# Scan and two feed-forward layers on one core: the narrow tile moves to the front, the opening, the output copies, the weight roundings and the gate's affine step are reordered

## What is computed

```python
# x, f_logit: (2, 6080, 256); lower_bound: (256,)
f = lower_bound + (1.0 - lower_bound) * sigmoid(f_logit)
i = 1.0 - f
for t in range(S):                      # per batch row and channel
    h = f[:, t] * h + i[:, t] * x[:, t]
    y[:, t] = h
# then, on the 12160 tokens, two layers one after the other:
h = x @ w_in                            # (tokens, 256) @ (256, 2048)
g = h - np.tanh(h)                      # layer 2: g = np.maximum(0.01 * h, h)
out = g @ w_out                         # (tokens, 2048) @ (2048, 256)
```

## Time and profile before

| | us |
|---|---|
| median of 3 runs | 2082.29 (2079.81 to 2082.47) |
| profiled execution, its own time | 2082.31 |
| its span, first to last instruction | 2080.5 |
| PE busy | 2020.8 (97%) |
| DVE busy | 1626.4 (78%) |
| ACT busy | 1225.4 (59%) |
| POOL busy | 101.8 (5%) |
| mean granted TensorE clock | 0.995 of full |

### The profile page before, as it was taken

How to read it: one execution, slowest core, us unless ns; L and a number is a source line. 1 busy time by engine, 2 the same in 40 slices (tenths; PEclk the granted TensorE clock), 3 DMA queues, 4 the chain that set the end, 5 groups by cost and what they waited for, 6 DMA issues and landing times.

```text
span 2080.5 us, 28416 instructions
## 1 busy us (share of the span) xinstructions
PE 2020.8 (97%) x8700; PEld 1628.8 (78%) x8700; DVE 1626.4 (78%) x2511; ACT 1225.4 (59%) x2168; POOL 101.8 (5%) x101
## 2 busy tenths in 40 slices
PE   6899999999999999999989999999999999999999
PEld 4678778787787877878878778787787877877888
DVE  7888888888888888888787776777777767777676
ACT  4576766766767667676664554544545545455454
POOL 3410000000000000000540000000000000000000
PEclk9999999999999999999999999999999999999999
DMA  3201101101011010010110100101101011010000
GB/s 112 71 31 31 50 14 57 40 20 54 26 40 40 20 60 30 28 58 20 56 64 1 41 21 20 40 0 40 40 0 40 0 40 40 0 40 18 20 21 18
DMA packets 38215, 71.13 MB, mean 34 GB/s; under 512 B 3360, under 2 KB 5920, under 8 KB 38176
## 3 DMA queue, kind: packets, MB, share of 16 engines
q1 hardware_dynamic: 38176, 70.66, 10.1%
HBM read 45.75 MB, written 24.90 MB: 34 GB/s over the span
## 4 chain that ended last, share of the span: by engine, by line
PE 89%; DVE 6%; ACT 3%; issue 2%; DMA 0%; SPq 0%; POOL 0%; ACTq 0%; DVEq 0%
PE y_ps L291 16%; PE y_ps L293 16%; PE y_ps L292 16%; PE x_ps L282 8%; PE x_ps L281 8%; PE x_ps L283 8%; PE q_ps L281 4%; PE q_ps L282 4%; PE q_ps L283 4%; DVE full L702 2%; PE p_ps L281 2%; PE p_ps L282 2%; PE p_ps L283 2%; DVE g_lo L719 1%; DVE part L689 1%
## 5 line engine op out<-in xcount | busy, mean ns | idle before, releaser
L291 PE MATMUL y_ps<-g_hi,wo_hi 128*128 128x512 f32 (+1 forms) x1536 | 610.4, 397 | 29.6 <-ACT y_out L499 18.9
L486 ACT CAST g_hi<-full 128x512 fp32r<-128x512 f32 (+1 forms) x768 | 473.1, 617 | 260.7 <-DVE full L702 135.2
L293 PE MATMUL y_ps<-g_hi,wo_lo 128*128 128x512 f32 (+1 forms) x1536 | 605.8, 394 | 0.0
L292 PE MATMUL y_ps<-g_lo,wo_hi 128*128 128x512 f32 (+1 forms) x1536 | 602.5, 392 | 0.0
L719 DVE TENSOR_TENSOR g_lo<-full,g_hi 128x512 fp32r<-128x512 f32 (+1 forms) x768 | 511.0, 686 | 116.1 <-ACT g_hi L486 110.9
L451 ACT COPY part<-x_ps 128x512 f32<-128x512 f32 (+1 forms) x576 | 334.2, 580 | 267.7 <-PE x_ps L283 257.7
L291 PEld LDWEIGHTS y_ps<-g_hi,wo_hi 128*128 128x128 f32 x1536 | 288.6, 188 | 108.5 <-ACT y_out L499 26.0
L293 PEld LDWEIGHTS y_ps<-g_hi,wo_lo 128*128 128x128 f32 x1536 | 289.4, 188 | 67.7
L292 PEld LDWEIGHTS y_ps<-g_lo,wo_hi 128*128 128x128 f32 x1536 | 288.8, 188 | 61.8
L281 PE MATMUL x_ps<-x_hi,wi_hi 128*128 128x512 f32 (+1 forms) x768 | 301.8, 393 | 24.0 <-POOL wi_lo L831 14.7
L282 PE MATMUL x_ps<-x_lo,wi_hi 128*128 128x512 f32 (+1 forms) x768 | 303.9, 396 | 0.0
(11 more groups left out here) (51 smaller groups left out, 1710.5 us busy)
## 6 DMA issues: line engine op xcount, KB each, us to landing
y<-y_out SPq DMA_DIRECT2D x22, 512.0 KB, 2.8
raw<-y SPq DMA_DIRECT2D x22, 512.0 KB, 4.1
out<-y_out SPq DMA_DIRECT2D x22, 512.0 KB, 2.8
gate<-f_logit SPq DMA_DIRECT2D x40, 256.0 KB, 2.7
drive<-x SPq DMA_DIRECT2D x40, 256.0 KB, 2.9
wi_stage<-w_in SPq DMA_DIRECT2D x16, 256.0 KB, 3.2
wo_stage<-w_out SPq DMA_DIRECT2D x16, 256.0 KB, 2.9
y_out<-f_logit SPq DMA_DIRECT2D x4, 256.0 KB, 4.1
```

Source lines behind the costliest of these rows:

```text
L291: nc.tensor.matmul(bank, hi, g_hi[:, g % 2, c, :W], start=start, stop=False, skip_group_check=True)
L292: nc.tensor.matmul(bank, hi, g_lo[:, g % 2, c, :W], start=False, stop=False, skip_group_check=True)
L293: return nc.tensor.matmul(bank, lo, g_hi[:, g % 2, c, :W], start=False, stop=stop, skip_group_check=True)
L486: nc.scalar.copy(g_hi[:, g % 2, c, :W], full[:, c, :W]).then_inc(g_hi_ready, 1)
```

## The change

1. **Narrow tile first.** The 448-token tile is now the first of each layer, tiles 0 and 12; tiles 11 and 23 have 512. Loops and special cases shift by one.
2. **Opening.** ScalarE takes the first three units, rounds the three plain weight blocks of group 0 that need no sum (`first_wi_round`), X11, the fourth unit, then the sums part; the three chain copies of slot 0 stand between the x roundings, in the order T2, copy, T3, T1, copy, X21, X22, copy, T4. PE has its own `first_slot`: X11 waits only for the first part of the weights, and T3 and T1 come ahead of X21. GpSimd splits group 0 in two parts. VectorE's splits follow the same order.
3. **Gate affine on ScalarE.** `forget_gate` is an Identity activation with scale and bias behind each squash; VectorE's line 608 is gone (44 instructions).
4. **Output copies.** The two `drain` of b=0 stand in slot 0 ahead of `bend` of C21 (in layer 2 ahead of `leak`). Those of b=1 stay in slot 1.
5. **Weight roundings.** `wi_round` stands ahead of `bend` of C11; `wo_round` stays after `round_g` of C11. In tile 0 GpSimd's order is `sum_weights(g+2)`, `wi_split(g+1)`, `wo_split(g)`.
6. **SBUF.** `carry` is allocated last and `zeros` before `bound`; `part`, `full`, `g_hi`, `g_lo`, `y_out` and `zeros` then start at multiples of 128 bytes.

The core of the diff (the transfers' addresses go through `tokens`, and the order of loop and written-out tiles follows from point 1):

```diff
-    W_LAST = seq - LAST * BANK
...
+    W_FIRST = seq - LAST * BANK
...
     def width(s):
-        return W_LAST if isinstance(s, int) and s % TILES == LAST else BANK
+        return W_FIRST if isinstance(s, int) and s % TILES == 0 else BANK
+
+    def tokens(t, b):
+        return b * seq if isinstance(t, int) and t == 0 else t * BANK - (BANK - W_FIRST) + b * seq
...
-        carry = sb("carry", [P, 4], F32)
         part = sb("part", [P, 2, 3, BANK], F32)
...
+        zeros = sb("zeros", [P, BANK], BF16)
         bound = sb("bound", [P, KD], F32)
...
-        zeros = sb("zeros", [P, BANK], BF16)
+        carry = sb("carry", [P, 4], F32)
...
+            def first_slot():
+                W = W_FIRST
+                chain, p_bank, q_bank = x_ps[:, 0, :W], p_ps[:, :W], q_ps[:, :W]
+                pe.wait_ge(first_wi_ready, 1)
+                pe.wait_ge(x_ready, 1)
+                product(chain, 0, W11, X11, W, True, False).then_inc(chain_done, 1)
+                pe.wait_ge(wi_ready, 1)
+                pe.wait_ge(x_ready, 2)
+                pe.wait_ge(chain_copied, 1)
+                product(chain, 0, S2, T2, W, False, False).then_inc(chain_done, 1)
+                pe.wait_ge(x_ready, 3)
+                pe.wait_ge(chain_copied, 2)
+                product(chain, 0, S3, T3, W, False, False).then_inc(chain_done, 1)
+                pe.wait_ge(x_ready, 4)
+                product(q_bank, 0, S1, T1, W, True, False).then_inc(q_done, 1)
+                pe.wait_ge(x_ready, 5)
+                product(p_bank, 0, W12, X21, W, True, True).then_inc(p_done, 1)
+                pe.wait_ge(x_ready, 7)
+                pe.wait_ge(chain_copied, 3)
+                product(chain, 0, W22, T4, W, False, True).then_inc(chain_done, 1)
+                pe.wait_ge(c22_ready, 1)
+                product(q_bank, 0, S4, X22, W, False, True).then_inc(q_done, 1)
...
+            def forget_gate(t, i):
+                W = width(t)
+                k = SCAN_ORDER[i] // 2
+                act.wait_ge(squash_ready, 4 * t + i + 1)
+                nc.scalar.activation(
+                    gate[:, i % 2, :W], gate[:, i % 2, :W], ACT.Identity,
+                    scale=gate_scale[:, k:k + 1], bias=gate_shift[:, k:k + 1],
+                ).then_inc(gate_ready, 1)
+
+            def first_wi_round():
+                act.wait_ge(wi_in[0], 16)
+                nc.scalar.copy(wi_hi[:, 0, W22:S1, :], wi_stage[:, 0, 1:4, :]).then_inc(first_wi_hi_ready, 1)
+
+            def first_wi_sums_round():
+                act.wait_ge(sums_w_ready, 1)
+                nc.scalar.copy(wi_hi[:, 0, S1:, :], wi_stage[:, 0, 4:8, :]).then_inc(wi_hi_ready, 1)
...
                 if scans and g in (1, 2, 3, 4):
                     squash(s + 1, g - 1)
-                copy_chain(q, par, 1, W)
+                    forget_gate(s + 1, g - 1)
+                if not begins:
+                    copy_chain(q, par, 1, W)
...
+                if first and g + 1 < GROUPS:
+                    wi_round(g + 1)
+                if isinstance(s, int) and s == LAST and g >= 1:
+                    wi_round(GROUPS + g - 1)
+                if isinstance(s, int) and s == SWITCH and g == 0:
+                    wi_round(2 * GROUPS - 1)
                 if layer == 1:
                     bend(s, g, C11, W)
...
                 if layer == 1:
                     bend(s, g, C22, W)
+                if g == 0 and not first:
+                    drain(s - 1, 0, 0)
+                    drain(s - 1, 0, 1)
+                if layer == 1:
                     bend(s, g, C21, W)
...
                 if layer == 1:
                     bend(s, g, C12, W)
-                if g == 0 and not first:
-                    drain(s - 1, 0, 0)
-                    drain(s - 1, 0, 1)
...
             def slot(s, g):
                 if s == 0:
-                    wo_split(g)
+                    if g + 2 < GROUPS:
+                        sum_weights(g + 2)
                     if g + 1 < GROUPS:
                         wi_split(g + 1)
-                    if g + 2 < GROUPS:
-                        sum_weights(g + 2)
+                    wo_split(g)
```

179 lines of the change are left out of this document (93 added, 86 removed).

## The result

The changed kernel takes **2010.23 us** (median of 4 runs, 2009.69 to 2011.36); the kernel before, run beside it, 2081.59 us (4 runs, 2079.81 to 2082.47). The ratio is 0.9659, with a 95% interval of 0.9642 to 0.9676.

The account below looks back on a forecast made before the run. PE (TensorE) was taken to bound the kernel. From 2080.5 us, - 13.4 - 0.6 + 0.8 - 21.9 - 6.5 - 11.7 gave 2027.2, plus 1.8 outside the span 2029 us, range 2018 to 2049.

Parts of the forecast that it names:

- Step 6: SBUF start places (homes): matmuls on g fall to the x spacing, 2.9 ns each over 24 a slot, gaining 11.7 us.
- the first rival: Moving the SBUF start places gives nothing, all else as forecast: 2041 us; chance 0.27.
- Step 1: Output copies, tiles 1 to 10: earlier b=0 copies cut the waits, stage 837.4 us, a gain of 13.4.
- The term for the third copy: First b=1 output copy, wanted by PE in slot 1: late, taken as 0.2 us a boundary, ends 0 and 0.6.
- Step 2: Output copies, layer 2, tiles 13 to 23: both pairs in time, stage 919.2 us, gain 0.6; tail grows by 0.8.
- Step 3: Opening and tile 0: tile 1 starts at 105 us in place of 126.91, a gain of 21.9 us.
- Step 4: Tiles 11 and 12, at the turn of layers: 167.2 us in place of 173.7, a gain of 6.5 us.
- Step 5: Gate affine moved to ScalarE: costs nothing under 0.5 us of cover; VectorE's freed 0.5 us hidden under PE in loops.
- The homes do nothing: Rival: new SBUF start places leave the matmul spacing as it was, all else as forecast, 2041 us; chance 0.27.
- Tile 0 slow: Rival: tile 0's seven slots take 86 to 90 us in place of 77, total 2041 or 2053 us; chance 0.10.
- More is gained: Rival: GpSimd's work lies beside idle VectorE time, tile 0 at 98, the turn at 162, total 2017 us; chance 0.05.
- the slow rival: Identity needs its own ScalarE table loads, over 2 us for PE in 44 slots, total 2119 us; chance 0.02.

Follow-up runs that it names:

- e1: The changed kernel with carry and zeros allocated at their old places, so part, full, g_hi, g_lo and y_out start 32 bytes further on; 2048.69 us.
- e4: The changed kernel with the two output copies of b=0 back at the end of ScalarE's slot 0; 2032.69 us.
- e16: The changed kernel with ScalarE's weight roundings back at the end of the slot and GpSimd's old order; 2014.42 us.
- e15: The changed kernel with forget_gate back on VectorE in all loops, the opening keeping it on ScalarE; 2013.87 us.
- e2: The kernel before with only carry allocated last and zeros moved ahead of bound; 2042.82 us.
- e3: TensorE alone, groups of 60 matmuls with varied operand starts and columns, moving blocks 2176 bytes apart; within 228.3 to 234.3 ns a matmul at 512 columns.
- e8: TensorE alone, 24 groups of 60 matmuls with varied operand places, most moving blocks 64 to 160 bytes short; within 228.3 to 234.3 ns at 512 columns.
- e11: TensorE alone, with cases where moving operand and weights share a remainder; 227 ns a matmul at 512 columns when matched, 232.4 to 233.4 otherwise.
- e9: The changed kernel with 32 bytes put in ahead of everything, weights and moving operands alike; 2008.16 us, one run.
- e13: The changed kernel with SP issuing load_wi(n + 1) ahead of load_wo(n) in tile 0; 2009.69 us.
- e14: The changed kernel with sum_weights last in GpSimd's order in tile 0; 2009.33 us.
- e17: The changed kernel with GpSimd's subtraction of wo_split done twice in tile 0; 2020.76 us, one run.

## Why the prediction was wrong, point by point

**Step 6, the homes, is the step that failed.** It costed the gain from the difference between x and g matmuls inside one slot, 2.9 ns over 24 matmuls, 11.7 us in all. By e1 it is 38.5 us: in a wide slot 45 matmuls lose 5.6 ns each, 0.253 us, in 168 PE-bound wide slots; that would be 42.5 us, and the narrow slots of 9.18 in place of 9.30 and shorter waits at a longer slot take a part back. The working took the x matmuls for undisturbed, and so took the fast neighbours as the floor. They stood in the same disturbed run, and their 230.5 ns was part of the effect. The rows themselves had a hint that I noted and laid aside, in the first rival: "x products themselves differ by place". The range did not contain a value for a gain larger than this difference, because only "0" and "2.9 to 3.7 ns" had been asked of the trace; the kernel before has no stretch at 226.7 ns from which it could have been read. It does have single steps of 226 or 227 ns, three in a slot, among others of up to 236; a reader who had asked for the steps one by one would have seen that the mean of the x matmuls was no floor. The cause too was named wrongly: it is not a multiple of 128 bytes, but how far the moving operand stands from the weights: all distances that are multiples of 512 bytes were fast, those of 32 and 128 slow.

The Trainium skill's figure in "SBUF — State Buffer", section "Specifications (TRN2)" (lines of 16 bytes) would have had the homes at nothing. The runs differ from it: 32 bytes, a multiple of 16, cost 38.5 us. Against the page, following the trace was right, and the trace even understated it.

**Step 1, copies of tiles 1 to 10.** Mechanism right, e4 shows 0.9 us for each boundary. The term for the third copy came out at 0.55 us, near the upper end of 0.6, not at 0.2. It was right for the slot it was worked out at: in e1, at 10.453, it is 0.20. At 10.20 it is 0.55, so this too goes back to step 6. What the sum also left out is that a stop costs more than its idle time of 0.22, since the matmul it holds and those behind it start further apart. (The stage's sum comes to 837.6, not 837.4; nothing hangs on it.)

**Step 2, copies of layer 2.** Right: slot 1 takes 10.20 us there, no wait is left, and the stage is bare slots at the new spacing (9.70 for the first and 87 x 10.20, 897.1 in all, against 897.12). The tail of 10.15 is as forecast.

**Step 3, opening and tile 0.** The order of events was right, the size short by 6.2 us. The second product came at 18.30 (17.5 forecast), the third at 20.25 (19.6), slot 1 at 28.57 (26.4). The last product came at 27.28 (25.4 forecast): PE waits 2.18 us for VectorE's `part`, behind a tanh difference that took 1.26 us beside GpSimd's `wi_split(1)`, against 0.61 alone; and the splits of x ahead of it had taken 0.87 each beside `sum_weights`. The last product itself then ran at the half clock, 1.29 us to the start of slot 1 where the others took 0.8. Slots 1 to 4 took 12.94, 11.20, 12.30 and 12.43 us, the upper end of 10.8 to 12.5, and slots 5 to 7 33.8 in place of 31. The lower bound by VectorE's load held; taking the value nearest to it was the mistake, since the same bound had been short by 1.7 us for the kernel before, and 10.8 + 1.7 = 12.5 was there to be taken. The half clock fell on needed work as forecast: once, from 26.29 for 6.8 us, in PE's wait for the last product, and with it the mean of 0.82 in slot 1; what it cost there no run separates.

**Step 4, tiles 11 and 12.** 167.17 against 167.2, but by errors that cancel. Tile 11 had its slots at 10.20 and lost 7.5 us to the late blocks, not 4.1; tile 12 ran its narrow slots at 9.30. Of the 6.5 us gained, the output copies give 2.3 (e4 needs 169.49 us for the two tiles) and the roundings 1.1 (e16, like for like). The spacing gives nothing: e1, without it, needs 166.65. The rest, some 3 us, goes with the wide and the narrow tile changing places, which was not undone by itself.

**Step 5, the affine.** Its cost of nothing was right. That its removal from VectorE would gain nothing was right only for slots of 10.453 us: e15 shows 3.6 us in all and 3.8 in tiles 1 to 10. The cover was counted at the old slot length although step 6 made it shorter.

**Rivals.** "The homes do nothing", held at 0.27, is refuted by e1 and e2. "Tile 0 slow" was half right, 82.7 us in place of 77 rather than 86 to 90. "More is gained" had the right total side for another reason. The table loads of the slow rival did not occur: the Identity takes 0.81 us in all 44 places.

Undone one by one, the parts give 38.5 (places), 22.5 (copies), 4.2 (roundings, with GpSimd's order) and 3.6 us (affine): 68.8 of the 71.4. They are not shares that add up: the opening with the narrow tile first was not undone by itself, and slot 1 of tile 0 alone starts 7.9 us earlier, at 28.57 in place of 36.46, which is more than the 2.6 us left over. What one part gives depends on the others, as the affine and the third copy show.

## What to carry to other kernels

Lay out weights and moving operands of 512-column fp32r matmuls so that all start at the same remainder by 512 bytes (at 448 columns this was no clear gain: 9.30 or 9.12 us a slot matched, 9.15 to 9.20 with operands 32 or 128 bytes off), and look at the start-to-start time of the matmuls, not at their busy share: a PE that is 100% busy hid 2.4% here. When a difference between neighbours in a trace is used to size a gain, ask whether the better neighbour is itself disturbed. And when one step of a sum shortens the period, cost the covers of all other steps at the new period.

## What the runs showed of the hardware

- 512-column fp32r matmuls start 226.7 ns apart when both operands begin at one remainder by 512 bytes and 228 to 234 ns in the mean otherwise (e3, e8 and e11 with TensorE alone; 230.8 to 233.3 in the kernels). Whether a distance of 256 bytes would do was not tried. The absolute place makes no difference (e9), nor the block of weights being the same each time.
- Operands out of place slow down the matmuls between them: with g alone off by 32 bytes all 45 of a slot average 232.3 ns, with g off by 128 bytes 230.8.
- At 448 columns matched operands have two spacings, 206.7 and 202.7 ns. The same PE program with the same places shows the first in the changed kernel and the second in e13, e14 and e17. An unmatched group of e8 has 206.7 too.
- A stop that its row calls 0.22 us idle costs 0.55 us of slot: 0.38 to the start, 0.11 to the next, and distances of 231 to 236 ns in places over the next twenty matmuls. In e1, at the slower spacing, the same stop costs 0.20.
- Beside a GpSimd instruction, VectorE's subtraction of two SBUF operands took up to 2.47 us in place of 0.61, while GpSimd's split took up to 3.03 in place of 2.07.
